# Gates and values by seven block products in place of eight, and the last 64 bias rows in four-row steps

## The reference

```python
# q, k, v: 4 batches, 8 heads, 576 rows, 64 columns
scores = scale * np.matmul(q, k.transpose(0, 1, 3, 2))
psi_rel = np.log1p(np.abs(rel)); psi_i = np.log1p(np.maximum(pos[:, None], 1.0))
h = np.maximum((psi_rel / psi_i)[..., None] @ w1 + b1, 0.0)     # 32 hidden
scores = scores + (h @ w2).transpose(2, 0, 1)[None]             # bias: 8 heads, 576 x 576
attn = softmax(scores); x = (attn @ v), heads side by side      # 2304 x 512
gate = 1.0 / (1.0 + np.exp(-(x @ w_gate)))                      # 512 x 1536
val = x @ w_val                                                 # 512 x 1536
out = (gate * val) @ w_out                                      # 1536 x 512
```

## Time and profile before

| | us |
|---|---|
| median of 3 runs (lowest, highest) | 795.73 (795.14, 796.69) |
| profiled execution, its own time | 794.48 |
| its span in the trace | 792.6 |
| PE busy | 770.5 |
| VectorE busy, ScalarE busy, GpSimd busy | 349.7, 345.3, 196.1 |
| granted TensorE clock, mean share of full | 0.998 |

### The profile page before, as it was taken

How to read it: one execution, slowest core, us unless ns; L and a number is a source line. 1 busy time by engine, 2 the same in 40 slices (tenths; PEclk the granted TensorE clock), 3 DMA queues, 4 the chain that set the end, 5 groups by cost and what they waited for, 6 DMA issues and landing times.

```text
span 792.6 us, 13855 instructions
## 1 busy us (share of the span) xinstructions
PE 770.5 (97%) x5308; PEld 641.4 (81%) x5308; DVE 349.7 (44%) x845; ACT 345.3 (44%) x684; POOL 196.1 (25%) x363
## 2 busy tenths in 40 slices
PE   7778999999999999999999999999999999999998
PEld 4336777777777777789889998998999899989996
DVE  7995777777777777625402220222022112302220
ACT  6996777667777677633312221222122112202210
POOL 0002666556545457768100000000000000000000
PEclk9999999999999999999999999999999999999999
DMA  5879333332432332224401001000200010000001
GB/s 137 197 187 200 78 100 83 80 95 64 123 75 71 78 82 59 66 82 121 132 28 54 1 1 55 25 1 14 67 1 0 17 64 1 1 26 14 1 1 40
DMA packets 86336, 49.92 MB, mean 63 GB/s; under 512 B 60160, under 2 KB 79744, under 8 KB 86272
## 3 DMA queue, kind: packets, MB, share of 16 engines
q1 hardware_dynamic: 85840, 48.96, 23.5%
q10 hardware_dynamic: 432, 0.09, 0.1%
HBM read 28.98 MB, written 9.44 MB: 48 GB/s over the span
## 4 chain that ended last, share of the span: by engine, by line
PE 85%; DMA 5%; DVE 3%; ACT 2%; POOL 2%; issue 1%; SPq 1%; ACTq 0%; POOLq 0%; DVEq 0%
PE f_ps L1080 19%; PE g_ps L1026 17%; PE u_ps L1026 16%; PE v_ps L1006 11%; PE so_ps L942 8%; PE ty_ps L955 4%; PE tx_ps L967 3%; DVE feats L726 3%; PE so_ps L937 2%; DMA bias<-bias_rows 2%; POOL w L527 2%; DMA x_raw<-in_w_out 1%; PE tx_ps L984 1%; PE v_ps L886 1%; PE ty_ps L896 1%; ACT feats L579 1%
## 5 line engine op out<-in xcount | busy, mean ns | idle before, releaser
L838 DVE TENSOR_TENSOR hid<-u_ps,sig 128x384 f32<-128x384 f32 x72 | 40.1, 557 | 243.4 <-PE u_ps L1026 243.4
L1026 PE MATMUL g_ps<-x_h,w 128*128 128x384 f32 x576 | 146.5, 335 | 0.0
L1026 PE MATMUL u_ps<-x_h,w 128*128 128x384 f32 x576 | 146.2, 334 | 0.0
L620 ACT ACTIVATE probs<-neg_scores,neg_max 128x576 f32<-128x576 f32 x144 | 111.1, 771 | 60.6 <-DVE neg_max L760 60.5
L510 POOL TENSOR_SCALAR probs<-probs,recip 128x512 f32<-128x512 f32 x128 | 88.6, 692 | 159.2 <-DVE recip L780 159.2
L1026 PEld LDWEIGHTS g_ps<-x_h,w 128*128 128x128 f32 x576 | 104.0, 188 | 0.8 <-POOL w L527 0.4
L1026 PEld LDWEIGHTS u_ps<-x_h,w 128*128 128x128 f32 x576 | 103.9, 188 | 0.5 <-issue 0.5
L688 ACT ACTIVATE h_h<-hid 128x384 fp32r<-128x384 f32 x72 | 37.9, 526 | 152.2 <-DVE hid L838 152.2
L1026 PE MATMUL g_ps<-x_l,w 128*128 128x384 f32 x288 | 96.3, 334 | 0.0
L1026 PE MATMUL u_ps<-x_l,w 128*128 128x384 f32 x288 | 96.2, 334 | 0.0
L760 DVE CUSTOM_DVE_ANT_0 neg_scores<-so_ps,bias 128x576 f32<-128x576 f32 x128 | 91.9, 755 | 5.4 <-PE so_ps L925 3.2
(11 more groups left out here) (92 smaller groups left out, 1147.5 us busy)
## 6 DMA issues: line engine op xcount, KB each, us to landing
bias<-bias_rows SPq DMA_DIRECT2D x12, 576.0 KB, 6.1
x_raw<-attn_transposed SPq DMA_DIRECT2D x6, 768.0 KB, 4.7
out<-out_sb SPq DMA_DIRECT2D x18, 256.0 KB, 2.0
q_raw<-in_q SPq DMA_DIRECT2D x32, 128.0 KB, 2.5
k_raw<-in_k SPq DMA_DIRECT2D x32, 128.0 KB, 2.5
v_main<-in_v SPq DMA_DIRECT2D x32, 128.0 KB, 2.3
w_raw<-in_w_gate SPq DMA_DIRECT2D x12, 256.0 KB, 3.0
w_raw<-in_w_val SPq DMA_DIRECT2D x12, 256.0 KB, 2.9
```

The costliest lines, as they stand in the source:

```text
L620: nc.scalar.activation(probs[s % RING][:, place, :], neg_scores[:, place, :], ACT.Exp, bias=neg_max[:, stat(s, place)], scale=-1.0, accum_ ...
L838: nc.vector.tensor_tensor(hid[f % 2][:, :], u_ps[f % 3][:, 0:CH], sig[f % 2][:, :], ALU.mult).then_inc(gated, 1)
L1026: last = nc.tensor.matmul(bank[f % 3][:, 0:CH], w[:, f, part, i, t, :], x[:, t, :], start=m == 0, stop=m == len(terms) - 1)
```

## The change

**Products.** A chunk is now 768 tokens (`CHUNK`), three of them. A quad is two feature tiles by two blocks of 384 tokens by two halves of the inner dimension, of the gate (even number) or the value (odd number). Its four output blocks come from seven block products in place of eight, over sums of the inputs: x parts A11, A12, A22, S1 to S4 and weight parts B11, B21, B22, T1 to T4. A product is 6 matmuls (2 inner tiles by 3 terms) of the same form as before, 128x128 by 384 columns. Four of them are summed in one PSUM bank (`z_ps`: P1, P6, P7, P4), and ACT copies the bank out after the first, second and third (`keep_sum`) before PE adds the next; DVE adds two PSUM banks to these copies (`sum_block`).

There are 36 quads, 12 to a chunk. After every six quads (a phase, half of the features) PE makes the outputs of six token tiles by 18 matmuls each. ACT keeps the first phase's sum in `out_sb` and DVE adds the second's.

**Weights.** The split weights don't stay: every chunk loads them again, 512 KB a quad in `w_stage`, into two buffers of parts `wc`. For each quad POOL makes the sums (`sum_w`: 512, 256 and 256 elements a partition) and one low part (TA, 512), ACT the four high parts (512, 512, 512, 256), DVE three low parts (B1 512, TB 512, B22 256). TB, two of the weight sums, is the one in the title.

**x.** The first chunk's sums and parts are made by POOL during attention (`first_x`, 29 instructions); the later ones at the chunk's end by DVE (sums and four low parts), ACT (high parts) and POOL (three low parts).

**Bias.** The last 64 rows are taken in steps of four rows (`TAIL_STEP`) from a table of their own, `tail_win`, one transfer of 583 KB more, and each of the two tail duos is stored by four transfers in place of eight.

```diff
-TAIL_DMAS = 8
+TAIL_DMAS = 4
+PRODUCTS = {"P1": ("A11", "B11", "Z", True), "P2": ("A12", "B21", "X", True), "P6": ("S2", "T2", "Z", False),
+            "P5": ("S1", "T1", "Y", True), "P7": ("S3", "T3", "Z", False), "P4": ("A22", "T4", "Z", False),
+            "P3": ("S4", "B22", "Y", False)}
-        EARLY_GATES = {STEPS - 1: 0, STEPS: 1, STEPS + 1: 2}
+        X_LOAD_AT = SPP * 2 * HP + 4
+        EARLY = {STEPS - 1: ("P1", "P2"), STEPS: ("P6", "P5"), STEPS + 1: ("P7",)}
...
+            load_w(2)
             store_x(PAIRS - 1, 1)
...
+            sp.wait_ge(valued, 2 * PAIRS)
+            load_wo(0)
...
+            for n in range(QUADS):
+                c = n // (2 * PHQ)
+                if n + 3 < QUADS:
+                    load_w(n + 3)
+                if n == 1:
+                    load_wo(1)
```

On POOL, after attention:

```diff
+            for n in range(1, QUADS):
                 for piece in range(3):
+                    sum_w(n, piece)
+                low_w(n, "TA")
+                if n == PHQ:
+                    for f in range(HFT, FT):
+                        split_wo(f)
```

On ACT:

```diff
+            for n in range(QUADS):
+                if inside:
+                    keep_sum(n - 1, "P7")
+                if more:
+                    high_w(n + 1, "B1")
+                if n:
+                    keep_sum(n, "P1")
+                if inside:
+                    block(n - 1, "22")
+                if more:
+                    high_w(n + 1, "TA")
+                if inside:
+                    block(n - 1, "21")
+                if more:
+                    high_w(n + 1, "TB")
+                block(n, "11")
+                if n:
+                    keep_sum(n, "P6")
+                if inside:
+                    block(n - 1, "12")
+                if more:
+                    high_w(n + 1, "B22")
+                if n in WO_QUADS:
+                    for f in WO_QUADS[n]:
+                        split_wo(f)
```

On DVE:

```diff
+            for n in range(QUADS):
+                if inside:
+                    sum_block(n - 1, "22")
+                if values:
+                    hidden(n - 1, "22")
+                    hidden(n - 1, "21")
+                    low_h(n - 1, "22")
+                sum_block(n, "11")
+                if n % 2:
+                    hidden(n, "11")
+                if inside:
+                    sum_block(n - 1, "12")
+                if values:
+                    hidden(n - 1, "12")
+                    low_h(n - 1, "21")
+                if n % 2:
+                    low_h(n, "11")
+                if 1 <= n < QUADS - 1:
+                    low_w(n + 1, "B1")
+                if n < QUADS - 1:
+                    low_w(n + 1, "TB")
+                if values:
+                    low_h(n - 1, "12")
+                if n < QUADS - 1:
+                    low_w(n + 1, "B22")
```

On PE:

```diff
+            for n in range(QUADS):
+                if n:
+                    product(n, "P1")
+                if inside:
+                    product(n - 1, "P4")
+                if n:
+                    product(n, "P2")
+                if inside:
+                    product(n - 1, "P3")
+                if n:
+                    for name in ("P6", "P5", "P7"):
+                        product(n, name)
+                if n % PHQ == PHQ - 1:
+                    outputs(ph, 0, (0, 1, 2, 3))
+                    product(n, "P4")
+                    product(n, "P3")
+                    outputs(ph, 1, (0, 1, 2, 3))
+                    for i in range(2):
+                        outputs(ph, i, (4, 5))
+                    for i in range(2, OT):
+                        outputs(ph, i, tuple(range(HFT)))
```

More of the change, by code:

```diff
@@ new lines, in high_h, with block, split_wo @@
+            def high_h(n, b):
+                act.wait_ge(hid_done[b], n // 2 + 1)
+                act.wait_ge(out_summed, n // PHQ * OT)
+                nc.scalar.activation(h_block(h_h, n, b), block_tile(hid, b), ACT.Copy).then_inc(h_high[b], 1)
+            def block(n, b):
+                if n % 2:
+                    high_h(n, b)
+                else:
+                    sigmoid(n, b)
+            def split_wo(f):
+                if f == 0:
+                    act.wait_ge(wo_in[0], 16)
+                nc.scalar.activation(wo_h[:, f, :], wo_whole[:, f, :], ACT.Copy).then_inc(wo_high[0], 1)
@@ new lines, in _ @@
+            for n in range(QUADS):
+                c, at = divmod(n, 2 * PHQ)
+                inside = n % PHQ > 0
+                more = 1 <= n < QUADS - 1
+                if inside:
[23 more added lines that the diff above has]
+                if n % PHQ == PHQ - 1:
+                    keep_sum(n, "P7")
+                    for b in ("22", "21", "12"):
+                        block(n, b)
+                    if at < PHQ:
+                        for i in range(OT):
+                            keep_out(c, i)
+                    elif c + 1 < CHUNKS:
+                        for k in ("A11", "A12", "A22", "S1", "S2", "S3", "S4"):
+                            split_x(c + 1, k)
@@ new lines, in sum_x @@
+            def sum_x(c, k):
+                one, two, op = {"S1": (x_stage[:, 0, :, :], "A22", ALU.add), "S2": ("S1", "A11", ALU.subtract),
+                                "S3": ("A11", x_stage[:, 0, :, :], ALU.subtract), "S4": ("A12", "S2", ALU.subtract)}[k]
+                if k == "S1":
+                    for part in x_in:
+                        dve.wait_ge(x_in[part], 16 * (c + 1))
+                if k == "S2":
+                    dve.wait_ge(x_sum["S1"], c + 1)
+                if k == "S4":
+                    dve.wait_ge(x_sum["S2"], c + 1)
+                product = [p for p in PRODUCTS if PRODUCTS[p][0] == k][0]
+                dve.wait_ge(summed[product], 2 * PHQ * c)
+                one, two = (x_value(of) if of in X_PARTS else of for of in (one, two))
+                nc.vector.tensor_tensor(x_value(k), one, two, op).then_inc(x_sum[k], 1)
@@ L1075, in outputs @@
                 rows = slice(i * P, (i + 1) * P)
-                terms = [(hh, ww, t) for t in range(FT) for hh, ww in ((h_h, wo_h), (h_h, wo_l), (h_l, wo_h))]
+                terms = [(hh, ww, t) for t in tiles for hh, ww in ((h_h, wo_h), (h_h, wo_l), (h_l, wo_h))]
                 for m, (hh, ww, t) in enumerate(terms):
-                    if i == 0 and m == len(terms) - 3:
-                        pe.wait_ge(h_ready, c * FT + FT)
-                    last = nc.tensor.matmul(f_ps[i % 2][:, 0:DM], hh[:, t, rows], ww[:, t, :],
-                                            start=m == 0, stop=m == len(terms) - 1)
@@ L1082, in outputs @@
-                last.then_inc(out_summed, 1)
-            for c in range(CHUNKS):
-                for f in range(FT):
-                    if c > 0 or f not in EARLY_GATES.values():
-                        gate_part(c, f, 0)
-                    gate_part(c, f, 1)
-                if c == 0:
-                    pe.wait_ge(x_ready[1], PAIRS)
-                for i in range(OT):
-                    outputs(c, i)
+                    last = nc.tensor.matmul(f_ps[i % 2][:, 0:DM], hh[:, t, rows], ww[:, half * HFT + t, :],
+                                            start=t == 0 and m == 0, stop=t == HFT - 1 and m == len(terms) - 1)
```

651 lines of the change are left out of this document (414 added, 237 removed).

## The result

The changed kernel takes 777.1 us (median of 4 runs, 771.83 to 777.8) against 795.43 for the kernel before beside it (794.28 to 796.69): a ratio of 0.9755, 95% interval 0.9733 to 0.9776. The forecast was 763, so the gain came, 18 us, and 14 us of what was expected did not. The profiled execution took 776.97 us, its span is 775.1, and the sum of the forecast was 760.4 for that span: **14.7 us are to be found.** They are those of one execution: the fourth run took 771.83.

The account below looks back on a forecast made before the run. PE, busy 97% of the span, was taken as the bound. The terms 342.3 + 404.4 + 4.8 + 1.6 + 1.5 + 1.0 + 1.8 + 3.0 gave a 760.4 us span, 762.3 with 1.9 around it, forecast as 763, range 752 to 781.

Parts of the forecast that it names:

- rival A: Steady quads: DVE and POOL together set the pace, 7.82 us a quad, 779 us; chance 0.24 between the forecast and that.
- Part 1: PE's matmuls: 404.4 us after attention in place of 442.0, and 1.0 us less inside attention's last steps.
- Part 2: Bias tail: fewer store issues remove ACT's and DVE's waits, 3.1 us, and 0.9 of half clock; 4.0 us together.
- rival C: Bias tail: the last store lands as late and DVE's wait stays, 767 us; chance 0.58 together with the forecast.
- Part 3: POOL's new work in attention costs 0, ends 0 and 2 us; the burst of loads is covered.
- (a): Start of the layer: P4 of quad 0 waits 1.8 us for ACT's copy after P7.
- (b): Start of the layer: quad 3's weights, loaded behind w_out's first half, come late; 0.4 and 2.6 us lost.
- Part 5: Steady quads: PE sets 7.29 us each, other engines below; 1.5 us lost in all, plus 1 us for splitting w_out.
- The row against it: DVE and POOL exclude each other: 7.82 us a quad by whole records, 6.7 with overlaps; the second was taken.
- Part 6: Phase ends lose 0.3 us each at worst, 1.8 together; chunk ends are hidden; the tail stays 3.0 us.
- Rival B: Weight work becomes a closed circle, 9.4 us a quad, 826 us; slower from 8.4; chance of slower 0.04.
- Rival D: Start of the layer: loads come sooner and nothing is lost there, 753 us; chance 0.08 for under 757.

Follow-up runs that it names:

- z4: Changed kernel with z2's five moves and ACT's and DVE's splits of w_out's first half in quads 2 to 5 as one, two, one, two: 764.2 us, ratio 0.9616.
- x2: Changed kernel with POOL's six splits of w_out's second half held until phase 0's low parts are done, beside the outputs: 769.84 us, ratio 0.9681.
- x3: Changed kernel with ACT's and DVE's splits of w_out's first half in quads 3 and 5 (four, two), not 2, 3 and 4: 777.58 us, ratio 0.9783.
- x4: Changed kernel with ACT's copy of P7 moved ahead of the last attention result, and quad 3's weights loaded before w_out's first half: 773.99 us, ratio 0.9736.
- y1: Changed kernel with the second table's load (583 KB) issued behind the stores of the first three duos: 777.22 us, ratio 0.9757.
- z3: Changed kernel with z2's five moves and ACT's and DVE's splits of w_out's first half in quads 3 and 5, three each: 766.27 us, ratio 0.9642.
- x1: Kernel before with only the bias tail of the change: 795.03 us against 794.84, ratio 0.9996.
- z1: Changed kernel with POOL's 40 attention instructions placed anew, no 512-wide subtraction sharing a step with a piece of x: 774.71 us, ratio 0.9747.
- y2: Changed kernel with extra unread matmuls on PE, four behind each of the last ten bias units and eight behind the last: 784.9 us, ratio 0.9862.
- y4: Changed kernel with the low parts of TB's two weight sums moved from DVE to POOL: 803.32 us, ratio 1.0099.
- y3: Changed kernel without seven of POOL's 29 instructions on x in attention, PE's work kept the same: 772.82 us, ratio 0.9715.
- z2: Changed kernel with five moves together, those of y1, z1, x4 (two) and x2: 767.24 us, ratio 0.9644.

## Why the prediction was right, and where it was not

It was right in sign and in the largest terms, and 14 us too low: 777.1 lies in the range of 752 to 781, near its upper end. That it lies inside is in part luck: the upper end was rival A's, a slower steady quad, which did not come, and the 14 us are other losses, five terms too low and one 3.3 us too high.

**Part 1, right.** Product 1.04 us, output matmul 0.227, steady quad 7.29. The 1.0 us from fewer early matmuls is there too, won at the end of attention.

**Part 2, wrong in size.** The mechanism is as told: issues 5.65 us, DMA engines full afterwards (1.03 from 40 to 50 us), ACT's waits gone (but for z4), DVE's wait between 0.2 and 0.7 us or none. In the profiles with the new tail and neither disturbance the first values come 1.9 to 2.2 us earlier than before (x2, x3, x4, y1, z3) or 1.3 (z4); the forecast had 4.0. The step that failed is the addition: ACT's waits, DVE's wait and the clock behind it were summed as if each stood on the chain alone, and the earlier trace rows gave the half clock of one execution as a property of the kernel. The changed kernel's own profile had a longer one, with no wait of PE over 0.9 us before it from 60 us on, and ten of the 13 profiles with the new tail have none. In the medians (x1) nothing is left: rival C's outcome, but not C's mechanism, as the last store did land earlier.

**Part 3, wrong.** "Its normalisations are used two steps later, so I take 0": the slack of POOL's results was asked for, not who can be held while POOL works. A subtraction of 1.3 us that comes second in its step lies on DVE's addition, and behind that are the reciprocal, the next maximum and PE: 2.4 us, the upper end of 2 passed (z1 wins 1.5 of them back). The burst of loads was covered, as told.

**Part 4, (a) right, (b) and the dip too high.** The copy of P7 cost 1.60 us (1.8 forecast), quad 2 cost 1.03 in place of 3.0, and none of these waits brought a half clock in this profile (1.6 forecast). In y2's the same first wait, 1.60 us at 360 us, was followed by one, 0.61 and 0.54 in the windows from 360 to 364 us. The forecast's price came from a single wait of 1.7 us; of 28 such waits in all profiles three were followed by the half clock. With both orders changed (x4) both waits are gone.

**Part 5, right for the quads, wrong for w_out.** The row against it was decided rightly. By whole records the pair would need 7.82 us a quad; 7.29 was measured, so rival A did not come. With the Trainium skill's rule ("SBUF — State Buffer", section "Who interferes with whom"), that the loser is fully blocked for the whole instruction, the trace agrees as to the hold (a product of 0.56 us took 1.70 beside POOL), and as to "the whole instruction" not quite: that product ended 0.42 us behind POOL's record, 0.14 less than its own 0.56. Whether the pair stays under 7.29 because of such overlaps, or because not every instruction meets one of the other engine, no run tells apart. w_out's splits were put down at 1.0 us "beside 7.29 already used to 5.9 and 5.7": a busy sum against a period. What counted was the order: DVE's two splits stand ahead of the sum of block 22 that PE wants, and POOL's sums stretch the pair from 1.4 us (twice 0.69) to 2.4, hence 3.9 us:

```profile
369.07 2.36 DVE L1053 TENSOR_TENSOR wo_l<-wo_whole,wo_h 128x512 fp32r<-128x512 f32 x2
371.35 0.54 DVE L1032 TENSOR_TENSOR sig<-y_ps,keep 128x384 f32<-128x384 f32 x1
```

**Part 6, the step that cost most.** "0.3 us lost each time at worst" counted DVE's chain at its bare 0.56 us each, though the earlier trace rows had shown 1.00 for it beside POOL, and never asked what POOL does at the end of phase 0. The six splits of POOL are in the change and in no term of the sum. In the profiled execution they cost 3.2 us, less what DVE's chain costs anyway, and, by the clock, 2.8 more. x2 shows both gone; y1 to y4 show that the same order can also cost 1.9 us and no half clock. The later phases lose little; at the two chunk ends DVE's sums of x hold its addition of an output, 1.1 us each, "hidden" in the forecast.

**Rival B was nearer than 0.04 suggests.** A circle of its kind exists, and its point of decision, 8.4 us a quad, fits: with one low part of 1.3 us more on POOL (y4) a pair of quads took 17.0 us, 8.5 each, and the kernel was slower than before. In y4 it closes through POOL and ACT, without DVE's TB that B had in it. What kept the changed kernel off it is TB's low part on DVE ("The change" says that TB is in the title; it is not there). The forecast counted it in DVE's 5.7 us and never asked what its place is worth. Rival D, nothing lost at the start, did not come either; z4's 764.2 us are near the forecast's 763 by luck: z4 has none of the waits on `keep` for which the forecast counted 6.4 us with their clock.

## What to carry over

When two engines exclude each other, cost every instruction on the critical chain at its price beside the other engine, and go through the phases one by one: a steady state with room says nothing of the ends, where the chain is bare and one-time work (here w_out) tends to be put. Ask of a helper engine not only when its results are wanted, but whom it holds meanwhile, even an instruction of two columns. A term taken from one dip of the clock is a chance and not a price.

## What the chip showed that was not expected

- DVE's addition to 2 columns, 0.17 us alone, took 0.92 and 1.09 us behind POOL's subtraction of 512: it ended 0.01 and 0.03 us after POOL's record.
- The clock fell to 0.50 at PE's waits of 2.3 us and more at 386 to 405 us each time (the changed kernel, x3, x4, z1, z3), at one of 1.9 us there in y1 and y4 and not in y2 and y3. Of 28 waits of 1.6 to 1.7 us in the 14 profiles it fell at three: the one of the kernel before at 73 us, x2's at 319 and y2's at 360. The same waits in other kernels went by without a fall. At 69 us (the changed kernel, z1, z2) it fell in a stretch in which PE had waited 0.67 us, a wait that x2, z3 and z4 have too, without a fall.
- The first 32 bias matmuls take 2.3 to 2.4 us in some executions and 3.7 in others of like code, groups of four 0.48 in place of 0.29 us apart, with a granted clock of 1.00 in both kinds (slow in the changed kernel, x1, z1 and z2). In y2, y3 and y4 they are slow too, and there the granted clock was 0.50 for about three microseconds. What causes either stays open. The window of y3:

```profile
9.00:11.00 2.00, 2.00 (x20) 0.86 (x16) 1.55 (x4) 1.50 (x2) 0.00 (x0) 0.50 0.11 43
```
